# Moving an 8-byte tensor behind the activations, and placing four activations 0, 64, 128 and 256 bytes past the weights' grid

## What is computed

```python
qn = q / (norm(q, axis=1) + 1e-6); kn = k / (norm(k, axis=1) + 1e-6)   # over the 6016 rows
a  = softmax(kn^T @ qn / tau)            # 256 x 256 for each batch
x  = v @ a                               # 12032 x 256
x2 = (sigmoid(x @ w_gate) * (x @ w_val)) @ w_out          # d_ff 1536
h  = x2 @ w2_in;  out = (h - tanh(h)) @ w2_out            # d_ff 2048
```

## Time and profile before

| | |
|---|---|
| median of 3 runs | 2411.64 us (2408.39 to 2413.62) |
| the profiled execution | 2413.12 us, span 2411.3 us |
| granted TensorE clock, mean | 0.994 |
| TensorE busy, matmul | 2370.7 us, 98% of the span |
| weight loads busy | 1932.8 us, 80% |
| VectorE busy | 1164.3 us, 48% |
| ScalarE busy | 936.6 us, 39% |
| GpSimd busy | 105.3 us, 4% |
| DMA | 61.81 MB, mean 26 GB/s |

### The profile page before, as it was taken

One profiled execution on the slowest core, in us unless ns is written; L12 is line 12 of the kernel. 1 busy time (PEld: TensorE's weight loads), 2 busy tenths in 40 slices (PEclk: granted clock), 3 DMA queues, 4 the chain that ended last, 5 costly groups with the idle time before them and its releaser, 6 DMA issues.

```text
span 2411.3 us, 28301 instructions
## 1 busy us (share of the span) xinstructions
PE 2370.7 (98%) x10332; PEld 1932.8 (80%) x10332; DVE 1164.3 (48%) x1643; ACT 936.6 (39%) x1550; POOL 105.3 (4%) x76
## 2 busy tenths in 40 slices
PE   7899999999999999999989999999999999999998
PEld 6778888888888888888888888888888888888888
DVE  7965445445344454453554544534434445445444
ACT  4544334334344343343433433433434334334343
POOL 3450000000000000000130000000000000000000
PEclk9999999999999999999999999999999999999999
DMA  9720000100100001001110010010010000100000
GB/s 296 227 62 6 13 9 9 17 9 9 17 9 9 14 3 17 9 7 17 27 44 16 2 16 9 9 17 9 9 17 9 9 11 7 17 9 7 9 9 7
DMA packets 211649, 61.81 MB, mean 26 GB/s; under 512 B 200224, under 2 KB 200480, under 8 KB 211616
## 3 DMA queue, kind: packets, MB, share of 16 engines
q1 hardware_dynamic: 208304, 49.31, 9.5%
q0 software_dynamic: 3312, 12.06, 1.6%
HBM read 49.02 MB, written 12.32 MB: 25 GB/s over the span
## 4 chain that ended last, share of the span: by engine, by line
PE 94%; issue 2%; DVE 1%; POOL 1%; SPq 1%; DMA 1%; ACT 1%; DVEq 0%; ACTq 0%
PE up L752 55%; PE acc L752 22%; PE x_acc L752 17%; DMA qk_in<-in_k 1%; DVE sq_sum L536 1%; POOL in_w_lo L382 0%; PE x_acc L778 0%; POOL out_w_lo L382 0%; SPq L304 0%; ACT squares L399 0%; SPq L294 0%; POOL in_w_hi L380 0%; POOL out_w_hi L380 0%; DVE vt_lo L627 0%; DVE g_lo L651 0%
## 5 line engine op out<-in xcount | busy, mean ns | idle before, releaser
L444 ACT ACTIVATE func_out<-up 128x512 f32<-128x512 f32 (+1 forms) x672 | 396.4, 590 | 871.3 <-PE up L752 871.3
L651 DVE TENSOR_TENSOR g_lo<-product,g_hi 128x512 fp32r<-128x512 f32 (+1 forms) x672 | 468.7, 697 | 403.8 <-ACT g_hi L452 403.4
L452 ACT ACTIVATE g_hi<-product 128x512 fp32r<-128x512 f32 (+1 forms) x672 | 418.5, 623 | 451.4 <-PE acc L752 233.3
L642 DVE TENSOR_TENSOR product<-up,func_out 128x512 f32<-128x512 f32 (+1 forms) x288 | 196.2, 681 | 484.5 <-ACT func_out L444 484.3
L645 DVE TENSOR_TENSOR product<-up,func_out 128x512 f32<-128x512 f32 (+1 forms) x384 | 261.2, 680 | 197.9 <-ACT func_out L444 189.7
L752 PE MATMUL up<-x_lo,in_w_hi 128*128 128x512 f32 (+1 forms) x768 | 300.7, 392 | 1.0 <-DVE x_lo L634 1.0
L752 PE MATMUL up<-x_hi,in_w_lo 128*128 128x512 f32 (+1 forms) x768 | 300.5, 391 | 0.0
L752 PE MATMUL up<-x_hi,in_w_hi 128*128 128x512 f32 (+1 forms) x768 | 300.4, 391 | 0.0
L752 PE MATMUL acc<-g_lo,out_w_hi 128*128 128x512 f32 (+1 forms) x768 | 299.9, 390 | 0.0
L752 PE MATMUL acc<-g_hi,out_w_hi 128*128 128x512 f32 (+1 forms) x768 | 299.6, 390 | 0.0
L752 PE MATMUL acc<-g_hi,out_w_lo 128*128 128x512 f32 (+1 forms) x768 | 299.6, 390 | 0.0
(11 more groups left out here) (122 smaller groups left out, 2303.1 us busy)
## 6 DMA issues: line engine op xcount, KB each, us to landing
v_in<-in_v SPq DMA_DIRECT2D x176, 64.0 KB, 2.3
out_rows<-out_sb SPq DMA_DIRECT2D x176, 64.0 KB, 1.9
qk_in<-in_q SPq DMA_DIRECT2D x29, 384.0 KB, 4.1
qk_in<-in_k SPq DMA_DIRECT2D x29, 384.0 KB, 5.4
w_stage<-in_moe_w_out POOLq DMA_DIRECT2D x4, 512.0 KB, 4.2
w_stage<-in_moe_w_gate POOLq DMA_DIRECT2D x3, 512.0 KB, 5.0
out_sb<-in_moe_w_val POOLq DMA_DIRECT2D x3, 512.0 KB, 4.2
out_sb<-in_moe_w_out POOLq DMA_DIRECT2D x3, 512.0 KB, 4.2
```

What stands on the lines that cost most here:

```text
L444: act.activation(func_out[:, half, cut], src[:, cut], func).then_inc(func_made, 1)
L452: act.activation(hi[:, i % SLOTS, cut], product[:, half, cut], ACT.Copy).then_inc(g_hi_made, 1)
L642: dve.tensor_tensor(product[:, half, cut], up[2 * (i % 2) + 1][:, cut], func_out[:, half, cut], ALU.mult).then_inc(prod_made, 1)
L651: dve.tensor_tensor(lo[:, i % SLOTS, cut], product[:, half, cut], hi[:, i % SLOTS, cut].bitcast(F32), ALU.subtract).then_inc(g_lo_made, 1)
```

## The change

tau_inv is made after the activations in place of before v_in. The activations are made in another order, with pads that nothing reads or writes: func_out, product, vt, 64 bytes, g1, 64 bytes, x2, 128 bytes, g2, tau_inv. What is computed, the instructions of every engine, their order and their semaphores stay as they were.

```diff
         ident = sb("ident", [P, P])
         ones = sb("ones", [P, P])
-        tau_inv = sb("tau_inv", [P, 2])
         v_in = sb("v_in", [P, KC, TB, Q])
...
-        x2_hi, x2_lo = pair("x2", [P, KC, T])
-        vt_hi, vt_lo = pair("vt", [P, KC, T])
-        g1_hi, g1_lo = pair("g1", [P, SLOTS, T])
         func_out = sb("func_out", [P, 2, T])
         product = sb("product", [P, 2, T])
+        vt_hi, vt_lo = pair("vt", [P, KC, T])
+        sb("pad_g1", [P, 16])
+        g1_hi, g1_lo = pair("g1", [P, SLOTS, T])
+        sb("pad_x2", [P, 16])
+        x2_hi, x2_lo = pair("x2", [P, KC, T])
+        sb("pad_g2", [P, 32])
         g2_hi, g2_lo = pair("g2", [P, SLOTS, T])
+        tau_inv = sb("tau_inv", [P, 2])
```

## The result

The changed kernel takes 2389.06 us (2385.13 to 2389.86, 4 runs) against 2412.39 us (2408.39 to 2413.62): a ratio of 0.9903, 95% interval 0.9886 to 0.992. It is faster by 1%; 2.7% was forecast. The profiled execution is one of 2385.13 us with a span of 2383.3.

A forecast was written before the change was run, and what follows sets the result against it. TensorE-bound: 408 matmuls a tile, 0.2333 us between starts. Savings of 60.2 us (512 columns) plus 5.1 (384 columns) make 65.3, from 2413.1 to 2347.8, stated as 2347; range 2277 to 2394 at 0.80, likeliest 2343 to 2353.

The forecast's parts named there:

- (1): Queues: moving the 8-byte tensor brings everything behind it down 32 bytes; no wait, instruction or order changes.
- (3): ScalarE and VectorE on the moved tensors: at most 1% faster, beside TensorE's work; slack taken under 0.1 us, so zero.
- (5): Batch change: TensorE's 6.20 us stall stays, hanging on GpSimd's work; a shift may give or take 3 us.
- step (4): First 142 us (gram, loads, folds of batch 0): zero change, with 1.5 us (1%) either way.
- step (2): Matmuls streaming vt, g1, x2, g2: all get the fold's 0.2267 us; 60.2 us for 512 columns, 5.1 for 384.
- (d): 384-column matmuls before batch 1's folds: 0.1767 us, 424 cycles; read as 17/16 cycles a column plus 16 for 32 bytes off.
- (c): Folds of batch 1, called the one place with both operands on the weights' grid: twelve in 2.72 us, 0.2267 us each.
- (b): Gram matmuls, float32, 256 columns: 0.2156 us each, losing almost nothing off the grid; only full-rate streams suffer.
- The first, vt alone: Rival: only distance 0 is cheap, so vt alone gains 23 us, giving 2390; chance 0.14, including vt and one more.
- The second (distance helps): Rival: 64 or more bytes part weight loads and stream, down to gram's 0.2156 us; 134 us, giving 2279; chance 0.14.
- the fourth: Rival, the slow side: cost grows with distance from the weights, +128 us, giving 2541; chance 0.13.
- The third: Rival: place matters not at all, the folds are quick for something else; 2412 us, no effect; chance 0.07.

The follow-up runs named there:

- mixed kernels: Three kernels against the kernel before, pads giving the streams of one stretch two distances from the weights modulo 512: 2375.34, 2366.59 and 2377.12 us.
- the first experiment: Against the kernel before, only the 8-byte tensor tau_inv moved behind the activations, their order kept and no pads: 2351.85 us, ratio 0.9761.
- the shifted kernel: Against the kernel before, tau_inv moved behind the activations and 32 bytes put ahead of the first weight, shifting weights too: 2348.38 us, ratio 0.9747.

## Why the prediction was right and wrong

**Right**: the bound and its kind, the direction, what a common distance of 0 is worth, and that no wait or other engine gets in the way. The steps (1), (3) and (5) stand. x2_hi takes 599 ns and x2_lo 692 (600 and 692 before), the room ahead of x2 is 1.24 us, the stall moved by 0.2 us. Of step (4) the zero stands but not its 1.5 us: the first matmul on vt starts 2.6 us earlier in the changed kernel's profile, and over all kernels this start lies anywhere in 10 us (last section). With all four at distance 0 the forecast's tile comes out, 92.48 us against 92.5, and its sum nearly: the medians differ by 2410.39 - 2351.85 = 58.5 us, the profiled executions by 63.9, where 65.3 were summed.

**Wrong: step (2)**, "I take the fold's price for all". It gave the places of g1 and x2 no price, and took for granted that a matmul's price doesn't hang on its neighbours'. Of the distances tried, the fold's price holds for 0 and 256 only, and only where no other distance shares the stretch. Worked out for a usual tile of the changed kernel:
- all at 0: 92.48 us.
- each at its own distance's price, vt 226.7, g1 (64) 228.9, x2 (128) 232.4, g2 (256) 226.7: 144 x 226.7 + 72 x 228.9 + 96 x 232.4 + 96 x 226.7 ns = 93.2 us. So 0.7 us go to the places of g1 and x2.
- measured: 94.10 us. The other 0.9 us go to mixing: in the first stretch 230.8 ns against the additive (144 x 226.7 + 72 x 228.9) / 216 = 227.4, in the second 230.5 against 229.5. The 230.8 is above the price of either of its two distances. The mixed kernels show such a surplus in each stretch that pairs 0 with 64 or 128, and next to none where it pairs 0 with 256.

Of the 2.72 us that distance 0 would bring a tile, 1.1 are left, and by 23.5 tiles' worth of columns that is 26 of the 28 us between the profiled executions; the earlier start has the rest. Why a distance has the price that it has stays open.

**The reason given under (d) was wrong too.** I split the 48 cycles in 17/16 a column and 16 for the place, from the two widths at distance 32. At distance 0 the 384-column matmuls, in the timeline of the kernel with the 8-byte tensor moved alone, show another split. The first two of these rows, thirteen intervals apart, stand ahead of the second fold of the batch change:

```profile
1209.86 0.33 PE L752 MATMUL acc<-g_hi,out_w_hi 128*128 128x384 f32 x1
...
1212.11 0.39 PE L752 MATMUL x_acc<-val_w_lo,att_t_hi 128*128 128x512 f32 x1
...
1213.50 0.39 PE L752 MATMUL x_acc<-val_w_lo,att_t_hi 128*128 128x512 f32 x1
...
1214.87 0.33 PE L752 MATMUL up<-x_lo,in_w_hi 128*128 128x384 f32 x1
```

2.25 / 13 = 173.1 ns is 415 cycles of 2.4 GHz, some 32 over 384, and 226.7 ns is 32 over 512. (These thirteen are the settled part of the 24 matmuls between two folds; the eleven ahead of them, from 1207.92 us, take 176 ns each.) So the loss at distance 0 is the same for either width; it does not grow with the columns.

Nor does 176.7 ns belong to distance 32. The trace of the kernel before has the same 18 matmuls of 384 columns, one chunk of U and one of D, at the same places in the last tile of batch 0 (the first two rows) and in that of batch 1 (the last two):

```profile
1195.10 0.34 PE L752 MATMUL up<-vt_lo,gate_w_hi 128*128 128x384 f32 x1
...
1198.28 0.34 PE L752 MATMUL up<-vt_lo,gate_w_hi 128*128 128x384 f32 x1
...
2342.21 0.34 PE L752 MATMUL up<-vt_lo,gate_w_hi 128*128 128x384 f32 x1
...
2345.33 0.34 PE L752 MATMUL up<-vt_lo,gate_w_hi 128*128 128x384 f32 x1
```

3.18 / 18 = 176.7 ns in the one and 3.12 / 18 = 173.3 in the other, 424 and 416 cycles, and so through the whole stretch. The second has no cost of place at all. What differs is around them (GpSimd is busy for 1.48 of the first 3.18 us and for none of the 3.12); which of it counts was not tried. So the 16 cycles for a place, and the 5.1 us for 384 columns, rested on one of two values that the trace held. The argument by which I held distance against the weights for unlikely ("the rest grows with the columns and so looks like the stream's own") had no ground.

**Under (c) and (b) the rows say less than I read.** The rows above also show the same fold as in the earlier trace rows, with the same operands at the same distance, at 2.76 us for its twelve where it took 2.72: the first six at 1.39 / 6 = 232 ns, the last six at 1.37 / 6 = 228. All six folds of this batch change take 2.76 us with the 8-byte tensor moved alone, and 2.76 in the changed kernel; in the kernel before the first took 2.77 and the other five 2.72. And these folds are not "the one place" with both operands at distance 0: those of batch 0 have them too, at the upper clock, and this one takes 2.30 / 10 = 230 ns:

```profile
106.04 0.40 PE L752 MATMUL up<-val_w_hi,att_t_hi 128*128 128x512 f32 x1
...
108.34 2.75 PE L778 MATMUL x_acc<-qk_in 128*128 128x256 f32 x12
```

So the distance alone does not fix a matmul's price. The mixed kernels show that the matmuls before it count; that they are what makes the difference between these folds is argued, not shown. I had read one row as the price of a place, and that this row's 226.7 is what long stretches at distance 0 settle on was luck. The gram rows of (b) tell nothing of the place: both its operands lie in qk_in, the loaded and the streamed one, so their distance from each other is 0 whatever the grid, in the kernel before as in the changed one.

**The rivals.** The first, vt alone, named a total of 2390 and the measured one is 2389, yet it is not what happened: vt gained less than it said (its stretch is at 230.8), x2 and g2 gained too, and the sum agrees by chance. The second (distance helps) falls, since no distance tried came below 226.7 ns, and the fourth (cost in proportion to distance, 2541) with 256 bytes at 226.7. The third falls with the first experiment. So does, for this kernel, what the prediction took from the rule of the Trainium skill on 16-byte lines (SBUF — State Buffer, Specifications), that 32 bytes off is as good as 0. Its other rule, a read port each for weight loads and the stream (same page, Who interferes with whom), does not by itself explain the shifted kernel, in which only the weights' place changed.

**Open.** What the two streams of reads share was not found. The prices nearly repeat after 256 bytes (0 and 256 both 226.7, 192 and 448 both 233.3, but 128 at 232.4 and 384 at 233.3), and no rule was found that gives them. Whether the weight in use counts, or the distance between successive weights, was not told apart either. It was not tried with weights that aren't loaded for each matmul. A pace that needs several matmuls to settle fits a coupling of the loads and the streams, but that is argued, not shown.

## What to carry to other kernels

Where float32r matmuls follow each other without a pause, look at the distance between starts, not at the busy share: 560 cycles for 512 columns in place of 544 was 2.4% of the kernel, and one 8-byte tensor ahead of the activations caused it. Put small tensors last and keep streamed operands and weights at the same place modulo 512; then measure, since pads chosen one by one took back more than half of the gain here. A price read from one row holds for the row's place and for what ran around it: read the same operation in all the places where it stands.

## What the runs showed that was not expected

At the lower clock level (a granted clock of 0.50 in these 1.71 us) the changed kernel's matmuls on vt, now at distance 0, take the same time as before at distance 32:

```profile
130.39 0.63 PE L755 MATMUL up<-vt_hi,gate_w_lo 128*128 128x512 f32 x1
...
132.10 0.63 PE L755 MATMUL up<-vt_hi,val_w_hi 128*128 128x512 f32 x1
```

Four intervals in 1.71 us are 427 ns, as in the earlier trace rows. The 16 cycles between these two distances are there at the upper level only; other distances were not seen at the lower.

The stretch ahead of the tiles differs from one profiled execution to the next: the first matmul on vt starts at 131.5 us in the kernel before, 128.9 in the changed one and at 125.8 to 135.8 in the others, with the same instructions. A difference of a few us between two kernels can lie there, and the usual tile, which repeats within 0.05 us in the traces of the kernel before, of the changed one and of the one with distance 0, is the better measure.
